# Decay table read from DRAM in 2 KB pieces and reordered on chip, query powers spread by a matmul, first chunk loads in another order

## The reference

```python
q, k, v: (2, 8, 768, 64), lam: (8,)            # batch, heads, sequence, head_dim
Dmask   = where(rel >= 0, lam ** rel, 0)       # rel = pos_i - pos_j
lam_pow = lam ** (pos + 1)
for each block:
    intra = ((qb @ kb.T) * Dmask) @ vb
    inter = (qb * lam_pow) @ kv_state
    out   = intra + inter
    kv_state = lam ** block * kv_state + (kb * lam ** (block - 1 - pos)).T @ vb
x = attention output as (2, 768, 512)
u = x + real(fft over sequence and hidden); ch = relu(norm(u) @ w1) @ w2; x2 = u + ch
out = (sigmoid(causal_conv5(x2)) * (x2 @ w_val)) @ w_out
```

## Time and profile before

| | us |
|---|---|
| median of 3 runs (lowest, highest) | 451.03 (449.82, 452.81) |
| profiled execution, its own time | 451.31 |
| its span in the trace | 449.5 |
| TensorE busy in the span | 434.8 (97%) |
| VectorE, ScalarE, GpSimd busy | 264.5, 150.2, 146.4 |

### The profile page before, as it was taken

The page is one execution under the profiler, slowest core; times in us unless marked ns, Lnnn a source line. Parts: engine busy times, 40 slices in busy tenths (PEclk is TensorE's granted clock), DMA queues, the critical chain, the costliest instruction groups (busy, mean ns, idle before and its releaser), DMA issues.

```text
span 449.5 us, 7168 instructions
## 1 busy us (share of the span) xinstructions
PE 434.8 (97%) x2934; PEld 415.0 (92%) x2934; DVE 264.5 (59%) x433; ACT 150.2 (33%) x284; POOL 146.4 (33%) x97
## 2 busy tenths in 40 slices
PE   9799869899999999999999999999999999999997
PEld 8688769789999999999999999999999999889985
DVE  2446897978356944454424327948557548999220
ACT  1145342274212331113342227353124233515221
POOL 1334461158422222523539223234224251500000
PEclk9899989999999999999999999999999999999999
DMA  6968720224022030202112212012112110001112
GB/s 202 382 211 273 206 79 2 65 59 158 2 93 94 0 95 1 93 1 94 55 41 95 54 41 93 29 66 95 34 61 93 32 63 2 1 1 70 71 47 93
DMA packets 13889, 36.52 MB, mean 81 GB/s; under 512 B 1561, under 2 KB 3105, under 8 KB 13857
## 3 DMA queue, kind: packets, MB, share of 16 engines
q1 hardware_dynamic: 13856, 36.07, 24.0%
HBM read 32.91 MB, written 3.15 MB: 80 GB/s over the span
## 4 chain that ended last, share of the span: by engine, by line
PE 85%; DVE 9%; DMA 2%; issue 2%; ACT 1%; SPq 1%; DVEq 0%
PE ps L532 10%; PE ps L534 10%; PE ps L555 10%; PE ps L533 10%; PE ps L554 10%; PE ps L553 10%; PE ps L644 2%; PE ps L643 2%; PE ps L642 2%; PE ps L621 2%; PE ps L622 2%; PE ps L623 2%; PE ps L406 2%; PE ps L489 2%; DMA chunks<-in_qkv 2%
## 5 line engine op out<-in xcount | busy, mean ns | idle before, releaser
L728 ACT ACTIVATE hh<-ps 128x384 fp32r<-128x384 f32 x64 | 31.5, 493 | 176.8 <-PE ps L534 176.8
L992 DVE SCALAR_TENSOR_TENSOR hl<-ps,hh 128x384 fp32r<-128x384 f32 x64 | 35.3, 556 | 87.0 <-ACT hh L728 87.0
L532 PE MATMUL ps<-cen_h,w1h_a 128*128 128x384 f32 x128 | 43.9, 343 | 0.5 <-DVE hl L992 0.5
L532 PE MATMUL ps<-cen_h,w1h_b 128*128 128x384 f32 x128 | 44.2, 345 | 0.0
L534 PE MATMUL ps<-cen_h,w1l_b 128*128 128x384 f32 x128 | 43.1, 337 | 0.0
L555 PE MATMUL ps<-hh,w2l_b 128*128 128x384 f32 x128 | 43.1, 337 | 0.0
L533 PE MATMUL ps<-cen_l,w1h_a 128*128 128x384 f32 x128 | 43.1, 337 | 0.0
L534 PE MATMUL ps<-cen_h,w1l_a 128*128 128x384 f32 x128 | 43.1, 337 | 0.0
L554 PE MATMUL ps<-hl,w2h_b 128*128 128x384 f32 x128 | 43.1, 337 | 0.0
L553 PE MATMUL ps<-hh,w2h_b 128*128 128x384 f32 x128 | 43.1, 337 | 0.0
L533 PE MATMUL ps<-cen_l,w1h_b 128*128 128x384 f32 x128 | 43.0, 336 | 0.0
(11 more groups left out here) (161 smaller groups left out, 1016.9 us busy)
## 6 DMA issues: line engine op xcount, KB each, us to landing
raw_a<-in_mlp SPq DMA_DIRECT2D x16, 512.0 KB, 4.7
raw_b<-in_mlp SPq DMA_DIRECT2D x16, 512.0 KB, 4.4
chunks<-in_qkv SPq DMA_DIRECT2D x12, 512.0 KB, 5.5
chunks<-in_qkv SPq DMA_DIRECT2D x22, 256.0 KB, 5.7
out<-out_sb SPq DMA_DIRECT2D x12, 256.0 KB, 2.0
raw_a<-in_val SPq DMA_DIRECT2D x2, 512.0 KB, 4.4
raw_b<-in_out SPq DMA_DIRECT2D x2, 512.0 KB, 4.4
seq_c<-const_seq SPq DMA_DIRECT2D x1, 768.0 KB, 6.0
```

Of the source, the lines that this page charges most:

```text
L532: mm(bank, wh_, xh, start=r == 0, stop=False)
L728: nc.scalar.activation(hh[:, slot, j], ps[j][:, 0:TB], ACT.Relu).then_inc(s_hh, 1)
L992: stt(hl[:, slot, j], ps[j][:, 0:TB], 0.0, hh[:, slot, j].bitcast(F32), ALU.max, ALU.subtract).then_inc(s_hl, 1)
```

## The change

It has four parts.

- **Layout.** `rv` now stands on 64 partitions (rows 0 to 31 all hold the even heads' powers, rows 32 to 63 the odd heads'), as position x 4 heads of one parity. The host hands over `lam` repeated in that form. The seven doublings cover 4 heads at a time on 64 partitions. Two of the rows are written to DRAM, 4 KB each.
- **Table.** It is read back in one transfer, one shifted run of 512 numbers (2 KB) for each partition and parity, into `shifted`, which lies in `out_sb`. `mask(0)` and `decay_keys(0)` read `shifted` as it is, 4 numbers from step to step. ScalarE copies it once into `decay` in the old order of heads, but forwards; all later chunks use that.
- **Query powers.** The two transfers into `qpow` are gone. TensorE spreads the powers over the partitions by two products with one row of the constant tile (`spread_powers`), and ScalarE copies the result from PSUM, reversed and scaled.
- **Order of loads, keep-warm products.** The values of chunk 0 are loaded ahead of the table; keys and queries of chunk 2 ahead of `hid_c`. The keep-warm products are 6, then 3 behind the spread, then 5 behind `scores(0)`.

```diff
-    H = lam.shape[0]
+    HP = lam.shape[1]
+    H = 2 * HP
...
-    WARM = 13
-    WARM_TABLE = 14
+    WARM = 6
+    WARM_POWERS = 3
+    WARM_TABLE = 5
...
-    rv_dram = nc.dram_tensor("powers_dram", (H, 2 * P), F32, kind="Internal").ap()
+
+    rv_dram = nc.dram_tensor("powers_dram", (2, 2 * P, HP), F32, kind="Internal").ap()
...
-            rv = probs[0:H, 0, 0:2].rearrange("h a t -> h (a t)")
...
-            qpow = small[:, 0:HP * (P + 1)].rearrange("p (a n) -> p a n", a=HP)
+            qpow = small[:, 0:HP * P].rearrange("p (a n) -> p a n", a=HP)
...
+        rv = zin[0:Dh].rearrange("p a r n -> p (a r n)").rearrange("p (i a) -> p i a", a=HP)
+        shifted = out_sb[:, :, :].rearrange("p e (i a) -> p e i a", a=HP)
...
-            sp.dma_start(rv[:, P - 1:P], lam.rearrange("(h a) -> h a", a=1)).then_inc(s_lam, 16)
+            sp.dma_start(rv[:, P - 1], lam).then_inc(s_lam, 16)
...
             load(0, 0, 2, s_tin)
             sp.wait_ge(s_pow, 2 + 7)
-            sp.dma_start(rv_dram, rv).then_inc(s_rv, 16)
+            sp.dma_start(rv_dram, rv[0:Dh:Dh // 2]).then_inc(s_rv, 16)
             load(0, 2, 3, s_kin)
+            load(0, 3, 4, s_vin)
             sp.wait_ge(s_rv, 16)
-            sp.dma_start(decay[:, :, :],
-                         bass.AP(tensor=rv_dram.tensor, offset=1, ap=[[1, P], [2 * P, H], [1, P]])).then_inc(s_tab, 16)
+            sp.dma_start(shifted[:, :, :, :].rearrange("p e i a -> p e (i a)"),
+                         bass.AP(tensor=rv_dram.tensor, offset=HP,
+                                 ap=[[HP, P], [2 * P * HP, 2], [1, P * HP]])).then_inc(s_tab, 16)
             load(1, 0, 2, s_tin)
-            load(0, 3, 4, s_vin)
-            for par in range(2):
-                sp.dma_start(qpow[par * Dh:(par + 1) * Dh],
-                             bass.AP(tensor=rv_dram.tensor, offset=par * 2 * P,
-                                     ap=[[0, Dh], [4 * P, HP], [1, P + 1]])).then_inc(s_tabq, 16)
             load(1, 2, 3, s_kin)
             load(1, 3, 4, s_vin)
+            load(2, 0, 2, s_tin)
             sp.dma_start(hid_c[:, :], hid_tab).then_inc(s_hid, 16)
-            load_chunk(2)
+            load(2, 2, 3, s_kin)
+            load(2, 3, 4, s_vin)
...
+            def spread_powers():
+                pe.wait_ge(s_pow, 2 + 7)
+                for par in range(2):
+                    row = slice(par * Dh // 2, par * Dh // 2 + 1)
+                    m = mm(ps[SIN][par * Dh:(par + 1) * Dh, 0:HP * P], ones[row, 0:Dh],
+                           rv[row, 0:P].rearrange("p i a -> p a i"), start=True, stop=True)
+                m.then_inc(s_spread, 1)
+
             pe.wait_ge(s_set, 1)
             keep_warm(WARM)
+            spread_powers()
+            keep_warm(WARM_POWERS)
             scores(0)
             keep_warm(WARM_TABLE)
...
-                    act.wait_ge(s_tabq, 32)
+                    act.wait_ge(s_qpow, 1)
...
                     nc.scalar.activation(state_l[:, hp], state[:, n % NC % 2, hp], ACT.Copy,
-                                         scale=qpow[:, hp, 0:1]).then_inc(s_sl, 1)
+                                         scale=qpow[:, hp, P - 1:P]).then_inc(s_sl, 1)
...
+            act.wait_ge(s_spread, 1)
+            nc.scalar.activation(qpow, ps[SIN][:, 0:HP * P].rearrange("p (a n) -> p a n", a=HP)[:, :, ::-1], ACT.Copy,
+                                 scale=float(D)).then_inc(s_qpow, 1)
+            act.wait_ge(s_tab, 16)
+            for par in range(2):
+                copy(decay[:, par::2, :], shifted[:, par, ::-1].rearrange("p i a -> p a i")).then_inc(s_dec, 1)
...
             nc.vector.memset(rv[:, P + 1:], 0.0).then_inc(s_pow, 1)
-            nc.vector.memset(rv[:, P:P + 1], 1.0).then_inc(s_pow, 1)
+            nc.vector.memset(rv[:, P], 1.0).then_inc(s_pow, 1)
             dve.wait_ge(s_lam, 16)
             for e in range(7):
                 w = 1 << e
                 if e:
                     dve.wait_ge(s_pow, 2 + e)
-                tt(rv[:, P - 2 * w:P - w], rv[:, P - w:P], rv[:, P - w:P - w + 1].broadcast_to([H, w]),
+                tt(rv[:, P - 2 * w:P - w], rv[:, P - w:P], rv[:, P - w:P - w + 1].broadcast_to([Dh, w, HP]),
                    ALU.mult).then_inc(s_pow, 1)
...
+                if n == 1:
+                    dve.wait_ge(s_dec, 2)
                 if n >= 2:
                     dve.wait_ge(s_pv, n - 1)
                 for par in range(2):
+                    weights = decay[:, par::2, :] if n else shifted[:, par, ::-1].rearrange("p i a -> p a i")
                     tt(probs[:, n % 2, par::2, :], ps[SCORE[par]][:, :].rearrange("p (a n) -> p a n", a=HP),
-                       decay[:, par::2, ::-1], ALU.mult).then_inc(s_pr, 1)
+                       weights, ALU.mult).then_inc(s_pr, 1)
...
-            pool.wait_ge(s_tab, 16)
...
+                if n == 0:
+                    pool.wait_ge(s_tab, 16)
+                if n == 1:
+                    pool.wait_ge(s_dec, 2)
...
-                tt(kd[:, :, :], kr[c], decay[:, :, 0:1].broadcast_to([P, H, Dh]), ALU.mult).then_inc(s_kd, 1)
+                pairs = lambda t: t.rearrange("p (a e) n -> p e a n", e=2)
+                last = pairs(decay[:, :, P - 1:P]) if n else shifted[:, :, 0].unsqueeze(3)
+                tt(pairs(kd[:, :, :]), pairs(kr[c]), last.broadcast_to([P, 2, HP, Dh]), ALU.mult).then_inc(s_kd, 1)
...
-                    pool.wait_ge(s_tabq, 32)
+                    pool.wait_ge(s_qpow, 1)
...
-                tt(qd[:, n % 2], qT[c], qpow[:, :, P - 1::-1], ALU.mult).then_inc(s_qd, 1)
+                tt(qd[:, n % 2], qT[c], qpow, ALU.mult).then_inc(s_qd, 1)
...
-    arrays = dict(in_qkv=np.stack([transposed(k), transposed(q), natural(k), natural(v)], 2), in_lam=inputs['lam'])
+    arrays = dict(in_qkv=np.stack([transposed(k), transposed(q), natural(k), natural(v)], 2), in_lam=np.repeat(inputs['lam'].reshape(H // 2, 2).T, Dh // 2, 0))
```

More of the change, by code:

```diff
@@ L63, in program @@
     R = D // P
-    HP = H // 2
     N = B * NC
@@ L166, in program @@
         s_lam, s_seq, s_hid, s_cw = (sem(n) for n in ("s_lam", "s_seq", "s_hid", "s_cw"))
-        s_pow, s_rv, s_tab, s_tabq, s_set = (sem(n) for n in ("s_pow", "s_rv", "s_tab", "s_tabq", "s_set"))
+        s_pow, s_rv, s_tab, s_spread, s_qpow, s_dec, s_set = (
+            sem(n) for n in ("s_pow", "s_rv", "s_tab", "s_spread", "s_qpow", "s_dec", "s_set"))
         s_tin = [sem(f"s_tin{c}") for c in range(RING)]
```

## The result

| | before | after |
|---|---|---|
| median of 11 runs each (lowest, highest), us | 451.37 (449.82, 454.26) | 449.51 (447.91, 450.80) |
| ratio, 95% interval | | 0.9954 (0.9933 to 0.9975) |
| profiled execution, its own time and span, us | 451.31, 449.5 | 449.47, 447.6 |

A forecast was written before the change was run, and what follows sets the result against it. TensorE is busy 97% of the span, so only the start's wait for chunk 2's keys and queries was left: 3.06 us earlier plus 1.61 for the clock, 4.7 in all, from 451.03 to 446.4 us; range 445.2 to 450.2.

The forecast's parts named there:

- Table and loads: Start: table there at 9.2 us; chunk 2's keys and queries landed at 13.7, with 3.60 MB moved, against 16.72.
- Powers: Doublings at the start: two shortest go, lengths 128 and 256 come, 0.40 us more, ending at 3.87.
- Write: Powers' write to DRAM, 8 KB in 2 pieces instead of 8: 0.1 us more than 1.35, landing at 5.3.
- Pieces: Table transfer in 2 KB instead of 512-byte pieces: passes in 1.35 us instead of 2.0 at 259 GB/s.
- The filled stretch: DMA from 5 to 7 us: filled by two loads queued ahead of the table, chunk 2's load lands at 12.9.
- Steps of 16 bytes: Reading 4 numbers apart: mask(0) 0.15 us more than 1.29; ScalarE's two copies 0.59 or 1.3 each, hidden.
- a rival of it: Slow spread: TensorE's rows read 4 numbers apart, taking 7.0 us; scores(2) at 17.4, total 450.0 us; chance 0.07.
- my series: Steps from table (9.2 us) through decay_keys(0), state_product(0), scores(1), from_chunk(0) and mask(1); scores(2) can start at 13.4.
- Spread: TensorE's spread of the query powers at the start: 1.74 us, from 3.9 to 5.7; hidden, or costs 0.5.
- the 12 us that I had named as a sign of being wrong: ScalarE's copies into decay: forecast to end at 10.4 to 11.8; ending behind 12 would show the prediction wrong.
- The clock: From scores(2) to scores(3): TensorE's clock no longer falls once the 2.31 us gap shrinks, gaining 1.61 us.
- The queue gives less: Rival: 5 to 7 us stays thin, all at 352 GB/s, chunk 2's load lands at 15.1; 447.8 us; chance 0.10.

The follow-up runs named there:

- f3: Changed kernel with 16 rows of 4 KB of powers written to DRAM instead of 2; the write took 1.91 us.
- e1: Kernel before with chunk 2's keys and queries issued ahead of the query-power transfers and hid_c; ratio to before 1.0017 (0.9988 to 1.0045).
- e3: Changed kernel with chunk 0's natural keys and values issued before the wait for the powers; ratio to before 0.9949 (0.9924 to 0.9973).
- g4: e3 with 12 instead of 5 keep-warm products behind scores(0); ratio to before 0.9946 (0.9921 to 0.9971).
- e2: Changed kernel with chunk 0's values moved back behind chunk 1's keys and queries; ratio to before 0.9974 (0.9950 to 0.9998).
- g1: Kernel before with chunk 0's natural keys and values issued before the wait for the powers; ratio to before 1.0057 (1.0031 to 1.0084).
- h2: Changed kernel's load order and spread without the 2 KB layout: powers written in eight 1 KB pieces, read in 512-byte pieces; ratio to before 0.9939 (0.9917 to 0.9960).

## Why the prediction was wrong

The step that failed is *Table and loads*, "I take 9.2" for the table and 13.7 for chunk 2's load. Measured: 12.1, and no wait for the load at all. By the bytes moved the load would be there at some 15.9 us, when my mark of 3.60 MB is passed. The table is late by 2.9 us: its transfer is issued 1.0 later than I had it and then takes 5.7 instead of 3.8. Point by point:

- **Powers.** 0.40 us more forecast, 0.43 measured (1.79 against 1.36). Right. But the load of the decays, for which I took nothing, at most 0.2, took 1.96 instead of 1.34: 0.62 missed. In the kernel before, the chain has

```profile
0.74 1.34 DMA probs<-in_lam
```

- **Write.** 0.1 forecast, 0.48 measured. The sum of these three put the table's issue at 6.38 instead of 5.36. The Trainium skill's rule that 2 rows run on 2 DMA engines (DMA: Bandwidth & Descriptors, "Why a DMA increments its semaphore by 16 and not by 1") is not tested by f3, whose 16 rows also leave 4 KB to each engine. The two packets did run side by side; each took 0.27 or 0.28 us, twice my estimate of 0.14, but most of the extra time lies ahead of them.
- **Pieces.** I put 0.65 us on 2 KB against 512 bytes. No row of the table above shows a gain. I had read the 259 GB/s from 7 to 8 us as the price of short pieces; but the changed kernel moves 219 and, with full engines, 243 GB/s from 7 to 11 us without any. So short pieces are not needed for a slow stretch. Its place in the start is not the whole reason either, since the kernel before moves 352 GB/s from 8 to 11 us; the cause stays open. My other slow row, 200 GB/s among the query powers, did go with those transfers (e1). The Trainium skill's lower bound of 512 B for line rate (same page, Specifications), which I set aside for that row, is borne out by the table of issue times.
- **The filled stretch.** I expected the two loads ahead of the table to fill the DMA engines from 5 us. I wrote myself that they stand behind SP's wait for the powers, and then did not move them: they are issued at 5.17, 1.3 us later than chunk 0's keys before, and from 5 to 7 us 69 GB/s pass instead of 175. The table comes 5.72 us after its issue, where I had 3.8. With nothing queued ahead of it the same transfer took 3.8 to 4.2 (e3, g4), so by this comparison the 0.52 MB of late loads cost some 1.7 us of it.
- **Steps of 16 bytes.** 0.15 us forecast for `mask(0)` from VectorE's 459 against 412 ns, 0.78 measured. The Trainium skill's sentence on lines of 16 bytes (SBUF — State Buffer, "Door 1: The DMA port swizzle") holds for VectorE and ScalarE, 1078 against 683 and 1122 against about 590 ns, and hardly for TensorE, 2.04 against 1.97 us at the low clock, where I had made a rival of it: that rival did not come. The slower `mask(0)` counts, since `scores(1)` waits for it (0.46 us "<-DVE probs L894"), a wait that my series left out.
- **Spread.** 1.74 us forecast, 2.04 measured, hidden under the table. Its two halves do overlap. ScalarE's copies end at 14.20; `mask(1)` starts at 15.55, so they stayed hidden, though behind the 12 us that I had named as a sign of being wrong.
- **The clock.** 1.61 us forecast, 1.54 measured, and shown by the four products in the kernel before. TensorE idles for 1.7 us and then twice for half a microsecond, and it holds in the profile; in e2's it fell behind a gap of 2.06 us. But a gap of that length does not always bring it down. In g1's profile `scores(2)` has the longest gap and takes 1.16 us, and the clock column stays at 1.00:

```profile
17.69 1.16 PE L406 MATMUL ps<-chunks 64*128 64x128 f32 x16 [2.46 <-DMA chunks<-in_qkv]
```

- **What stays.** Right: no later wait took the lead back.

In sum: the clock's 1.61 of the 4.7 was right; the 3.06 for the earlier `scores(2)` became -0.22, since the chain over the table, for which I had 13.4, came at 16.98. Of these 3.6 us 2.9 are the table's and 0.7 come behind it, most of them from `mask(0)`. Of the rivals, *The queue gives less* was nearest: it saw the thin stretch from 5 to 7 us, but priced only chunk 2's load by it and not the table.

## What to carry to other kernels

When a wait has two chains close behind each other (here the load at 16.7 and the table's `mask` chain at 14.8), a change that moves work from one to the other must price the second chain's every link by its new shape; a small transfer's own time is a link, too, and so is the time at which its issuer gets to it. A rate in one stretch of a trace is not yet the rate of the pieces in it; before it is put down to their size, look for a run with other pieces in the same place, and for one with the same pieces elsewhere. And try the cheapest cause first: four useless products gave 0.34%, the whole change 0.46%.

## What I had not expected of the hardware

- A load of 64 x 16 bytes took 1.96 us from issue to use and 8 x 4 bytes 1.34. 8 KB written from 2 partitions took 1.83 us in two pieces and 1.87 in eight (h2), and 1.35 from 8 partitions; 64 KB from 16 partitions took 1.91.
- In the start the DMA engines can be full and yet move far less than later: the changed kernel 243 GB/s from 8 to 11 us and 405 from 12 to 17, e3 293, 274 and 231 in the microseconds from 9 to 12 us and 389 and more from 13 to 17. The kernel before moved 352 from 8 to 11.
- Executions of one and the same kernel differ by some 4 us with the mean granted clock: 449.5 us near 0.996, 453.3 from 0.984 to 0.989. One fall of the clock, as from 17 to 21 us before, costs 1.5 to 1.6 us, nearly as much as the whole change gives.
